# Attention, an expert layer and a dense mixture layer on one core: the second layer takes its rows in expert order, half of them before the first layer ends

## What is computed

```python
def _moe_ref(x, modality_id, w_gate, modality_bias, w1, w2):
    logits = x @ w_gate + modality_bias[modality_id]
    e_idx = np.argmax(logits, axis=1)
    ...
    for e in range(E):
        mask = e_idx == e
        h = np.maximum(x[mask] @ w1[e], 0.0)
        out[mask] = gate_w[mask, None] * (h @ w2[e])

def _moe2_ref(x, w_gate, w1, w2):
    logits = x @ w_gate
    logits = logits - logits.max()
    P = np.exp(logits)
    for _ in range(8):
        P /= P.sum(1, keepdims=True) + 1e-09
        P /= P.sum(0, keepdims=True) + 1e-09
        P *= N / E
    for e in range(E):
        h = np.maximum(x @ w1[e], 0.0)
        out += P[:, e:e + 1] * (h @ w2[e])
```

## Time and profile before

| what | value |
|---|---|
| three timed runs, median (lowest to highest) | 1403.03 us (1402.81 to 1403.81) |
| profiled execution: time, span | 1405.03 us, 1403.0 us |
| PE busy | 1371.9 us, 98% of the span |
| DVE, ACT, POOL busy | 705.2, 450.6, 416.4 us |
| mean granted clock of TensorE | 0.994 of full speed |
| attention and routing | 0 to about 181 us |
| first layer's blocks | about 181 to 360.8 us |
| last block's product to the second layer's first product | 360.8 to 387.1 us |
| second layer | 387.1 to 1403.0 us |

### The profile page before, as it was taken

The page is one execution under the profiler, slowest core; times in us unless marked ns, Lnnn a source line. Parts: engine busy times, 40 slices in busy tenths (PEclk is TensorE's granted clock), DMA queues, the critical chain, the costliest instruction groups (busy, mean ns, idle before and its releaser), DMA issues.

```text
span 1403.0 us, 21674 instructions
## 1 busy us (share of the span) xinstructions
PE 1371.9 (98%) x7515; PEld 1221.7 (87%) x7516; DVE 705.2 (50%) x1290; ACT 450.6 (32%) x867; POOL 416.4 (30%) x615
## 2 busy tenths in 40 slices
PE   8999989999799999999999999999999999999999
PEld 7999678888688888999988889999888999988888
DVE  8886672141464644445454444455444445544444
ACT  6887432232243422223131222313122222322221
POOL 4111022222430523415052332505143241605330
PEclk9999999999999999999999999999999999999999
DMA  6440372121301011101110010011101011110001
GB/s 131 107 105 32 129 245 72 42 75 38 136 31 31 30 30 31 31 31 30 45 45 30 30 30 30 30 45 45 30 30 30 30 30 37 43 39 30 30 32 58
DMA packets 95647, 73.85 MB, mean 53 GB/s; under 512 B 43344, under 2 KB 76144, under 8 KB 95600
## 3 DMA queue, kind: packets, MB, share of 16 engines
q1 hardware_dynamic: 92560, 65.34, 15.5%
q0 software_dynamic: 2672, 7.88, 1.7%
q10 hardware_dynamic: 368, 0.02, 0.0%
HBM read 62.74 MB, written 10.49 MB: 52 GB/s over the span
## 4 chain that ended last, share of the span: by engine, by line
PE 92%; DVE 4%; ACT 1%; issue 1%; POOL 1%; DMA 1%; POOLq 0%; SPq 0%; DVEq 0%; ACTq 0%
PE ps L2025 37%; PE ps L2000 33%; PE ps L1886 5%; PE ps L1864 5%; PE ps L1684 3%; PE ps L1618 1%; PE ps L1644 1%; PE ps L1873 1%; PE ps L1630 1%; PE ps L1678 1%; PE ps L1798 1%; PE ps L1603 1%; PE ps L1693 1%; PE ps L1933 1%; PE ps L1844 0%
## 5 line engine op out<-in xcount | busy, mean ns | idle before, releaser
L2000 PE MATMUL ps<-x_hi,w_hi 128*128 128x384 f32 x896 | 301.7, 337 | 4.7 <-DVE x_lo L1447 3.8
L1529 DVE SCALAR_TENSOR_TENSOR acc<-ps,mix,acc 128x512 f32<-128x512 f32 x180 | 135.1, 751 | 329.2 <-PE ps L2025 329.2
L2000 PE MATMUL ps<-x_hi,w_lo 128*128 128x384 f32 x896 | 300.5, 335 | 0.0
L2000 PE MATMUL ps<-x_lo,w_hi 128*128 128x384 f32 x896 | 300.3, 335 | 0.0
L2025 PE MATMUL ps<-w_hi,h_hi 128*128 128x512 f32 x768 | 300.0, 391 | 0.0
L2025 PE MATMUL ps<-w_hi,h_lo 128*128 128x512 f32 x768 | 299.7, 390 | 0.0
L2025 PE MATMUL ps<-w_lo,h_hi 128*128 128x512 f32 x768 | 299.4, 390 | 0.0
L739 POOL TENSOR_TENSOR w_lo<-w_raw,w_hi 128x256 fp32r<-128x256 f32 x224 | 159.0, 745 | 89.5 <-ACT w_hi L934 89.5
L2000 PEld LDWEIGHTS ps<-x_hi,w_hi 128*128 128x128 f32 x896 | 168.9, 188 | 7.6 <-DVE x_lo L1447 4.2
L2025 PEld LDWEIGHTS ps<-w_hi,h_hi 128*128 128x128 f32 x768 | 144.1, 188 | 32.9 <-DVE h_lo L1489 5.0
L2025 PEld LDWEIGHTS ps<-w_hi,h_lo 128*128 128x128 f32 x768 | 144.1, 188 | 30.6
(11 more groups left out here) (280 smaller groups left out, 1781.4 us busy)
## 6 DMA issues: line engine op xcount, KB each, us to landing
w_raw<-in_moe_w_dram SPq DMA_DIRECT2D x64, 256.0 KB, 3.0
w_raw<-in_moe_w_dram SPq DMA_DIRECT2D x16, 1024.0 KB, 5.3
stage<-in_moe_w_dram SPq DMA_DIRECT2D x8, 1024.0 KB, 6.4
first_raw<-in_moe_w_dram SPq DMA_DIRECT2D x4, 1024.0 KB, 8.1
q_raw<-in_q_dram SPq DMA_DIRECT2D x12, 256.0 KB, 3.4
k_raw<-in_k_dram SPq DMA_DIRECT2D x12, 256.0 KB, 4.3
v_all<-in_v_dram SPq DMA_DIRECT2D x12, 256.0 KB, 4.4
x_rows_dram<-x_rows SPq DMA_DIRECT2D x12, 256.0 KB, 4.0
```

Of the source, the lines that this page charges most:

```text
L1529: dve.scalar_tensor_tensor(out=acc[:, m, :], in0=ps[:, 4 + t % 3, :], scalar=mix_flat[:, bass.ds(e + m * (E + 1), 1)], in1=acc[:, m, :], o ...
L2000: last = pe.matmul(ps[:, bank, 0:CT], w_part[:, j, w, ks], x_part[:, x, k, cols], start=(opens and k == 0 and n == 0), stop=(k == 1 and n ...
```

## The change

- **Order by expert.** Rows of the second layer stand in the order of the first layer's blocks, not of the tokens. A block is stored with a plain DMA at a row `row[b]`, the block's place without the padding before it; the next block overwrites the padding's rows. So a block's store waits, as before, for the one before it. DVE computes `row` (7 small ops) ahead of the first gate scaling, and the token's place (`token_places`, 8 small ops) in the last pair. POOL then writes the token numbers to `tokens_dram` (12 indirect DMAs of 4 bytes a row), SP reads them back (12 loads), and POOL, not SP, writes the output with indirect DMAs.
- **First half early.** Rows 0 to 767 are loaded by SP as soon as the stores of pair `last_pair - 3` are counted, into a buffer of their own (`y_early`). Their combinations stand on DVE between `split_next(last_pair, 0)` and `y_evacuate(last_pair, 0)`. Their 42 transposes are grouped by operand (`transpose_early(n)`, six each, in the order that the products want); the first three groups stand before `product2` of block 13, one behind it, three inside `up(0, 0, 0)`. Rounding and rests go by group, and each product of `up(0, 0, 0)` waits for its own operand alone. A group's rounding writes over `wsplit`, so it waits for block 13's product.
- **Weights.** The w1 sums and the first rests stand on POOL before the store of block 12, the second rests between the last two stores. ACT's `w1_round` stands before and behind `hT_round(last_pair, 1)`. w2 is still loaded behind the rows, now behind six tiles and not twelve, and is rounded in `up(0, 0, 1)`, one `up` later.
- **Idle transposes.** 14 and 90 become 4 and none.

```diff
+            half_done = sp.value_load(tab[0:1, TAB_H:TAB_H + 1], min_val=TILES - 3, max_val=MAXB - 3)
+            half_done = sp.snap(half_done >> 1, min_val=(TILES - 3) // 2, max_val=(MAXB - 3) // 2)
+            for c in range(2):
+                sp.wait_ge(y_buffer_free[c], half_done * 16)
+            for i in range(3):
+                for m in (i, i + 3):
+                    sp.dma_start(y_early[:, m, :], yd[:, m, :]).then_inc(y_loaded[i], 16)
             sp.wait_ge(y_stored, 1)
-            for i in range(TILES // 2):
-                for m in (i, i + TILES // 2):
-                    sp.dma_start(y_rows[:, m, :], yd[:, m, :]).then_inc(y_loaded[m], 16)
+            for i in range(3):
+                for m in (i + 6, i + 9):
+                    sp.dma_start(acc[:, m, :], yd[:, m, :]).then_inc(y_loaded[i + 3], 16)
             load_w2(0, 0)
...
# GpSimd
+            def store_y(i, c):
+                pool.wait_ge(y_copied, i * 2 + (c + 1))
+                pool.wait_ge(y_buffer_free[1 - c], i * 16 + (16 + 16 * c))
+                at_row = pool.value_load(row[0:1, bass.ds(i * 2 + c, 1)], min_val=0, max_val=N)
+                pool.dma_start(y_rows_dram[bass.ds(at_row, PART), :], y_blk[:, c, :]).then_inc(y_buffer_free[c], 16)
...
-            for c in range(2):
-                scatter_y(last_pair, c, last_pair * 4 + (c + 2))
-            pool.wait_ge(block_done, pairs * 2)
+            sums_w1(0, 0)
+            sums_w1(0, 1)
+            lows_w1(0, 0)
+            store_y(last_pair, 0)
+            lows_w1(0, 1)
+            store_y(last_pair, 1)
             pool.wait_ge(y_buffer_free[0], pairs * 16 + 16)
             pool.wait_ge(y_buffer_free[1], pairs * 16 + 16)
             hold(6).then_inc(y_stored, 1)
-            split_half(0, 0)
+            split_w2(0, 0)
             pool.wait_ge(local_max, 1)
             pool.partition_all_reduce(gmax[:, 1:2], gmax[:, 0:1], PART, REDUCE_MAX).then_inc(global_max, 1)
             split_half(0, 1)
+            pool.wait_ge(places_ready, 1)
+            for m in range(TILES):
+                pool.indirect_dma_start(out=tokens_dram, ..., in_=token_id[:, m:m + 1], in_offset=None)
...
# ScalarE
-            hT_round(last_pair, 1)
+            act.wait_ge(xr_loaded[0], last_pair * 16 + 32)
+            act.wait_ge(xr_loaded[1], last_pair * 16 + 16)
             w1_round(0, 0)
-            for i in range(3):
-                x2_round(i)
+            hT_round(last_pair, 1)
             w1_round(0, 1)
-            up_evacuate(0, 0, 0)
+            act.wait_ge(block_done, last_pair * 2 + 2)
+            for n in range(4):
+                early_round(n)
+            up_evacuate(0, 0, 0, after_p1=next_early, hook=lambda: early_round(6))
...
# VectorE
+            hT_rest(last_pair, 0)
+            split_next(last_pair, 0)
             for i in range(3):
                 x2_combine(i)
-            for i in range(3):
-                x2_rest(i)
+            token_places()
+            y_evacuate(last_pair, 0)
+            hT_rest(last_pair, 1)
+            y_evacuate(last_pair, 1)
+            for n in range(4):
+                early_rest(n)
+            up_finish(0, 0, 0, after_u2=lambda: early_rest(4), after_u3=lambda: early_rest(5),
+                      after_c11=lambda: early_rest(6))
             x2_combine(3)
-            up_finish(0, 0, 0)
...
# TensorE
             transpose_h(last_pair * 2 + 2)
-            keep_busy(14, 0)
+            pe.wait_ge(x2_combined, 3)
+            transpose_early(0)
+            transpose_early(1)
+            keep_busy(4, 5)
+            pe.wait_ge(hT_split, last_pair * 2 + 2)
+            transpose_early(2)
             product2(1, last_pair * 2 + 1, last_pair * 2 + 2)
-            keep_busy(90, 0)
-            for i in range(3):
-                transpose_y(i)
-            up(0, 0, 0)
+            pe.wait_ge(y_copied, last_pair * 2 + 2)
+            transpose_early(3)
+            up(0, 0, 0, behind={"P1": transpose_early_4, "P7": transpose_early_5, "P2": transpose_early_6})
```

More of the change, by code:

```diff
@@ L127, in attention_moe_moe @@
         idx_x = take("idx_x", [PART, 2], i32)
-        idx_y = take("idx_y", [PART, 2], i32)
+        token_id = take("token_id", [PART, TILES], i32)
+        place_f = take("place_f", [PART, TILES])
+        token_place = take("token_place", [PART, TILES], i32)
+        row_token = take("row_token", [PART, TILES], i32)
+        row_f = take("row_f", [PART, 24])
+        row = take("row", [PART, 24], i32)
         used = take("used", [PART, 1])
@@ L561, in _ @@
                 load_next_half(r, 1, r + 1, 0)
+            sp.wait_ge(tokens_placed, 16 * TILES)
+            for m in range(TILES):
+                sp.dma_start(row_token[:, m:m + 1], tokens_dram[m * PART:(m + 1) * PART, :]).then_inc(row_tokens_loaded, 16)
             load_next_half(E - 1, 0, E - 1, 1)
[L563 to L569, removed]
         @block.gpsimd
@@ L757, in _ @@
             split_half(0, 1)
+            pool.wait_ge(places_ready, 1)
+            for m in range(TILES):
+                pool.indirect_dma_start(out=tokens_dram,
+                                        out_offset=bass.IndirectOffsetOnAxis(ap=token_place[:, m:m + 1], axis=0),
+                                        in_=token_id[:, m:m + 1], in_offset=None).then_inc(tokens_placed, 16)
             with pool.Fori(0, E - 1) as r:
@@ L760, in _ @@
                 split_half(r + 1, 1)
+            pool.wait_ge(row_tokens_loaded, 16 * TILES)
+            for u in range(2, 4):
+                for t in range(6):
+                    m = tile_of(u, t)
+                    pool.wait_ge(out_bank_free, 24 * (E - 1) + u * 6 + t + 1)
+                    pool.indirect_dma_start(out=out,
+                                            out_offset=bass.IndirectOffsetOnAxis(ap=row_token[:, m:m + 1], axis=0),
+                                            in_=acc[:, m, :], in_offset=None).then_inc(out_stored, 16)
+            pool.wait_ge(out_stored, 16 * TILES)
         @block.scalar
@@ L956, in up_evacuate @@
                 act.activation(t_u2[:, g % 2, :], ps[:, 0, 0:CT], ACT.Copy).then_inc(p1_copied, 1)
-                w2_now = u % 2 == 0 and j == 0
+                if after_p1 is not None:
+                    after_p1()
+                w2_now = u % 2 == 0 and j == (1 if begin and u == 0 else 0)
                 if w2_now:
```

266 lines of the change are left out of this document (158 added, 108 removed).

## The result

| | before | after |
|---|---|---|
| timed runs, median (lowest to highest) | 1402.92 us (1402.79 to 1403.81) | 1394.83 us (1394.76 to 1395.04) |
| ratio, 95% interval | | 0.9938 (0.9924 to 0.9952) |
| span of the profiled execution | 1403.0 us | 1393.3 us |
| last DVE op ends, span's end behind it | 1400.60, 2.4 us | 1384.66, 8.6 us |

The change gained 8.1 us where 15.7 were forecast, and 1394.83 lies above the range, which ended at 1391.5. The second layer starts as early as forecast, but the kernel's end does not come as early.

The account below looks back on a forecast made before the run. PE bounds the kernel nearly everywhere, except 26.3 us between the layers. `down` earlier -16.3, output +0.5, one more op +0.1 sum to -15.7 us, off 1403.03: 1387.3 us, range 1381.5 to 1391.5.

Parts of the forecast that it names:

- the output's term: At the kernel's end: POOL's indirect stores instead of SP's stores cost +0.5 us, at most +4.
- one more op: Ahead of the routing table: one op more costs 0.1 us.
- DVE ahead of block 13's product: Before block 13's product: 12 slow combination ops and eight token ops on DVE make that product 4.4 us late.
- Rival (a): Before block 13's product: DVE ops don't pay POOL's price, product ends at 361.4, 4.2 us less, 1383; chance 0.15.
- Rival (d): Between the layers: the six early loads wait for the last blocks and the old gap stays; 1403; chance 0.01.
- Rival (b): Around block 13's product: PE's clock falls in the new wait, 1389.5; with a second fall at w2 1391; chance 0.3.
- 1.00 at 368: In the old gap between layers: full granted clock behind seven microseconds of transposes alone, cited against the skill's transpose rule.
- From the product to `down`: First product 1.95 us behind block 13's, at 367.5; 2.9 us wait for w2; `down` at 387.6, 16.3 us earlier.
- The token writes (c): Ahead of expert 1's sums: 12 indirect DMAs on POOL, forecast hidden at 12 us; rival +34 us, 1422, chance 0.02.

Follow-up runs that it names:

- e1_out_sp: The changed kernel, but SP writes the 12 output tiles with plain DMAs, in expert order, instead of POOL's indirect ones; 1389.29 us.
- e2_out_pool_plain: The changed kernel, but POOL writes the output tiles with plain DMAs, in expert order, instead of indirect ones; 1396.87 us.
- e5_pool_late_op: The changed kernel, but SP writes the output plainly and POOL issues only one 128x1 multiply that waits for the last DVE op; 1392.34 us.
- e4_out_split2: The changed kernel, but SP writes the last six output tiles plainly, POOL the six before indirectly, and POOL waits for nothing at its end; 1390.83 us.
- e7_combine_earlier: The changed kernel with the token ops moved into the second layer's first step and two combinations put ahead of block 12's rest on DVE; 1392.84 us.
- e3_out_wait_sp: The changed kernel, but the last wait, for all output stores, stands on SP and not on POOL; 1394.42 us.
- e9_w2_early: The kernel of e7_combine_earlier with w2 loaded once block 13's product is done and rounded from the first `up` on; 1388.82 us.
- e10_w2_early_wait_sp: The kernel of e9_w2_early with the last wait for the output on SP and not on POOL; 1387.52 us.

## Why the prediction was wrong, point by point

**The step that failed is the output's term**, "+0.5 us, at most +4". The sum took the end of the kernel to be the landing of the last store, and priced the move to POOL by how long a store takes to land. The landing was sized rightly: issue and landing took 3.0 us (1384.66 to 1387.7). Missing was what POOL does behind its last instruction, 5.2 us. The trace of before had it, hidden, on POOL at 1346.0, of the same length; a look at it would have shown that the term of 0.5 lacked something of 3.3 us at least, and the rows of DMAs could not show it. The tail grew by 6.2 us, 5.7 more than the sum held. That the time is POOL's and comes with any late instruction is shown by `e1_out_sp`, `e2_out_pool_plain`, `e5_pool_late_op` and `e4_out_split2`.

**The other 1.8 us** of the 7.5 by which the time missed: 0.3 is the last DVE op, 15.9 us earlier where the sum had 16.2 (16.3, less 0.1 for one more op). `down` did begin 16.3 us earlier; behind the w2 wait its first six matmuls took 1.66 us and not the 1.39 of before. The rest, 1.5, lies between spans and times: the sum went by the span of an execution that was 2.0 us above before's median; the changed kernel's profiled execution was at its median. Before's had the fall at 190, worth about those 2 us; whether its timed ones had it isn't shown. That the last DVE op met the forecast so closely is in part luck: 2.1 of its 15.9 us were there already at block 11's scaling (337.77, from 339.91), ahead of nearly all that the change moves, and the clock took 1.6 back in block 13's product.

**DVE ahead of block 13's product: right.** Combinations at 0.84 and not 0.87; token ops 3.1 us and not 2.7; the start at 342.09 and not 344.0, as block 12 came 2.2 us earlier and the step behind it took 0.3 us longer. The rest ended at 357.1 and not 359.1. Rival (a) falls: the pairing with POOL is real, 0.42 alone and mostly 0.84 to 0.96 paired in `e7_combine_earlier`. (The product end of 361.4 in that case is 361.2 by the sum's own terms.) Rival (d) falls too: the combinations did not wait for the early rows.

**Rival (b) came true, once, and did not decide.** Block 13's product took 7.37 us and not 5.5. Of these 1.9 us the clock's fall is 1.6, since without a fall the product took 5.73 to 5.75 us in the other kernels; the rest is the forecast's, as the product took 5.74 us before. The product had begun 2.0 us earlier than forecast, so the two cancelled, and 367.43 met the forecast 367.5 by two errors of opposite sign. The second fall, at the w2 wait, did not come in the changed kernel's profile, but did in `e4_out_split2`, the same kernel up to its output: its `down` began at 387.66 and its last DVE op ended 1.8 us later. Six kernels are the same up to the output, with the same waits within 0.05 us (1.96, 2.92 and 2.74 us). In block 13's product the clock fell in all but `e3_out_wait_sp`; at the w2 wait it fell in `e1`, `e2`, `e3` and `e4`, but not in the changed kernel and `e5`. So the length of these waits doesn't settle it, and what does is open. In `e9_w2_early` and `e10_w2_early_wait_sp`, where PE waits at most 0.63 us at the first place and 0.44 us at the second, neither fall came.

The Trainium skill, "TensorE: Matmul & The Clock Gate", section "Part 4: PE-mode transpose", says that a transpose does not count as PE-busy in the same way as a matmul. Read as "not at all", this does not agree with the trace of before: from 360.83 to 381 PE ran nothing but transposes, with pauses of up to 3.8 us, and the granted clock stayed at 1.00. The forecast's "1.00 at 368" alone is weak evidence for it, since the clock was 1.00 at 378 beside an idle PE as well.

**From the product to `down`: right.** 1.95 us to the first product, as forecast; `down` at 387.63 (387.6), with POOL's two w2 rests as the last wait, which held PE for 2.7 us (2.9). w2 landed 2.2 us later than the forecast 378: ACT waited 1.04 us for it, until 380.22. The forecast said that the wait would grow by as much; it did not grow, since ACT was held by the results of the products for the later chunks and reached the last two at 383.87 and 384.90.

**The token writes (c): right.** 12 indirect DMAs from 464.5, the first 1.30 and the others about 0.96 us each, with 0.3 between, 15 us; no wait of PE behind them. (By its own terms this rival gives a loss from 4.8 us each, not 4.9.)

## What to carry to other kernels

Before moving a last piece of work to another engine, look in the trace at what that engine does behind its last instruction, and let the engine with the dear end finish early. A path that is shortened ends at the next late operand: here the rounding of the weights. Moving it as well gave 3.5 us, wait and clock together, about as much as the 3.1 us of the token ops. Work moved ahead of one operand can delay another, as the combinations did with block 12's product. A gain or a loss of 2 us in one profiled execution can be one fall of the clock; look for the same fall in its neighbours before giving it to the change.

## What the runs showed of the hardware

- POOL's drain at the program's end took 5.21 us behind a wait and 4.46 us beside a small multiply. Where POOL's last DMA issue or its last operations still ran when it began, it took 5.2 to 6.4 us, and ended 3.3 to 5.2 us behind them. SP's, ACT's and DVE's took 0.01 to 0.62 us. PE's took 4.0 us, but began beside its last matmuls and was over before the last DVE op ended.
- An indirect store of 128 rows holds POOL for 0.96 us, a plain one for 0.54 to 0.59.
- A DVE op that adds two SBUF tensors of 128x256 took 0.42 us alone and mostly 0.84 to 0.96 beside POOL's sums. POOL's sums slowed as well: 0.72 to 0.75 us alone, mostly 0.80 to 1.03 beside DVE's.
- The clock's fall after the same waits came in one execution and not in another. A fall in block 13's product cost 1.6 us and the one at 190 1.9; with a fall at the w2 wait, the way from the first `down` to the last DVE op was 1.3 to 2.7 us longer than in the changed kernel.
